# Bonus sums of the first two chunks: two columns of u per head pair in 32-column strips, in place of 96 spread columns

## The reference, cut to what matters

```python
for t in range(S):
    cur = np.einsum('bhd,bhe->bhde', u[None] * kt, vt)
    y[:, :, t] = np.einsum('bhd,bhde->bhe', rt, state + cur)
    state = wt[:, :, :, None] * state + np.einsum('bhd,bhe->bhde', kt, vt)
```

## Time and profile before

| | us |
|---|---|
| median of three runs | 647.96 |
| the profiled execution | 647.89 |
| its span in the trace | 646.1 |
| PE busy | 639.0 (99%) |
| DVE busy | 418.1 (65%) |
| ACT busy | 238.2 (37%) |
| POOL busy | 295.6 (46%) |

### The profile page before, as it was taken

The page is one execution under the profiler, slowest core; times in us unless marked ns, Lnnn a source line. Parts: engine busy times, 40 slices in busy tenths (PEclk is TensorE's granted clock), DMA queues, the critical chain, the costliest instruction groups (busy, mean ns, idle before and its releaser), DMA issues.

```text
span 646.1 us, 13797 instructions
## 1 busy us (share of the span) xinstructions
PE 639.0 (99%) x5044; PEld 592.0 (92%) x5044; DVE 418.1 (65%) x786; ACT 238.2 (37%) x561; POOL 295.6 (46%) x370
## 2 busy tenths in 40 slices
PE   8999999999999999999999999999999999999998
PEld 5998999877788888999999999999999999999997
DVE  7888988965357666655565656565656565656564
ACT  4776555645445554222222222222222222222221
POOL 5897424420499999996019900019900019000000
PEclk9999999999999999999999999999999999999999
DMA  8953454300000133100012100012100011001011
GB/s 323 403 196 131 137 167 175 121 18 1 1 2 1 56 102 99 40 1 1 1 50 98 50 1 0 1 49 98 50 1 0 0 50 50 0 1 49 0 50 50
DMA packets 19043, 42.34 MB, mean 66 GB/s; under 512 B 2608, under 2 KB 8752, under 8 KB 18992
## 3 DMA queue, kind: packets, MB, share of 16 engines
q1 hardware_dynamic: 18704, 41.23, 18.5%
q10 hardware_dynamic: 288, 0.39, 0.2%
HBM read 37.16 MB, written 4.46 MB: 64 GB/s over the span
## 4 chain that ended last, share of the span: by engine, by line
PE 89%; POOL 5%; DVE 3%; issue 1%; DMA 0%; ACT 0%; POOLq 0%; DVEq 0%
PE bank L1351 29%; PE bank L1352 28%; PE bank L1353 28%; POOL w_lo L549 4%; PE bank L1197 1%; PE bank L1266 1%; DVE fr L870 1%; PE bank L1278 1%; DMA rkw<-rkw_dram 0%; DVE att L928 0%; DVE fr L889 0%; PE bank L1222 0%; POOL tok L530 0%; DVE bank L1001 0%; PE bank L1286 0%
## 5 line engine op out<-in xcount | busy, mean ns | idle before, releaser
L1351 PE MATMUL bank<-x_lo,w_hi 128*128 128x256 f32 (+2 forms) x416 | 138.2, 332 | 0.6 <-DVE w_lo L971 0.3
L1352 PE MATMUL bank<-x_hi,w_lo 128*128 128x256 f32 (+2 forms) x416 | 135.2, 325 | 0.0
L1353 PE MATMUL bank<-x_hi,w_hi 128*128 128x256 f32 (+2 forms) x416 | 135.2, 325 | 0.0
L1352 PE MATMUL bank<-w_hi,g_lo 128*128 128x384 f32 x384 | 129.6, 337 | 0.0
L1353 PE MATMUL bank<-w_hi,g_hi 128*128 128x384 f32 x384 | 129.3, 337 | 0.0
L1351 PE MATMUL bank<-w_lo,g_hi 128*128 128x384 f32 x384 | 129.0, 336 | 0.0
L833 ACT ACTIVATE g_hi<-bank 128x512 fp32r<-128x512 f32 x96 | 57.5, 599 | 144.3 <-DVE bank L1057 122.4
L1351 PEld LDWEIGHTS bank<-x_lo,w_hi 128*128 128x128 f32 x416 | 78.2, 188 | 10.6 <-issue 2.6
L1353 PEld LDWEIGHTS bank<-x_hi,w_hi 128*128 128x128 f32 x416 | 78.3, 188 | 7.4
L1352 PEld LDWEIGHTS bank<-x_hi,w_lo 128*128 128x128 f32 x416 | 78.3, 188 | 7.1
L1050 DVE TENSOR_TENSOR u_sum<-p_copy,bank 128x256 f32<-128x256 f32 x56 | 23.6, 421 | 92.1 <-ACT p_copy L757 91.4
(11 more groups left out here) (133 smaller groups left out, 1259.6 us busy)
## 6 DMA issues: line engine op xcount, KB each, us to landing
raw<-w_dram SPq DMA_DIRECT2D x48, 384.0 KB, 3.7
rkw<-rkw_dram SPq DMA_DIRECT2D x10, 772.5 KB, 4.5
tok<-tok_dram SPq DMA_DIRECT2D x10, 576.0 KB, 6.2
k_blocks_dram<-k_blocks SPq DMA_DIRECT2D x8, 256.0 KB, 4.1
kt_sb<-k_blocks_dram SPq DMA_DIRECT2D x32, 64.0 KB, 2.0
out_dram<-acc SPq DMA_DIRECT2D x10, 192.0 KB, 1.9
rkw<-rkw_dram SPq DMA_DIRECT2D x2, 512.0 KB, 4.5
rkw<-rkw_dram SPq DMA_DIRECT2D x2, 260.5 KB, 3.2
```

The costliest lines, as they stand in the source:

```text
L1351: pe.matmul(out, wh, ml, start=start, stop=False, skip_group_check=shared)
L1352: pe.matmul(out, wl, mh, start=False, stop=False, skip_group_check=shared)
L1353: return pe.matmul(out, wh, mh, start=False, stop=stop, skip_group_check=shared)
```

## The change

`u_blk` and `u_col` go, and with them the four activations on ACT and the semaphore `s_ub`. In their place stands `u_heads`, two columns for each head pair: the first head's u with zeros below, the second's with zeros above. The same two DMAs now write into it. PE's `bonus` takes for each pair four products with 32 tokens' columns of `rk` as weights and the two columns of `u_heads`; each gives 32 partitions of the bank. The bank thus holds each head's sum once (8 columns), and `bonus_v` reads it 48 times over through a broadcast.

```diff
-            u_col = sb("u_col", [P, PAIRS], scope=scope)
-            u_blk = sb("u_blk", [P, PAIRS, PD], scope=scope)
+            u_heads = sb("u_heads", [P, PAIRS, 2], scope=scope)
...
-        s_ub = sem("s_ub")
...
-        blocks = const[:, C_BLK:C_BLK + PD]
...
             for o in range(2):
-                u_heads = bass.AP(u_d.tensor, o * D, [[1, D], [PD, PAIRS]])
-                sp.dma_start(u_col[64 * o:64 * o + D, :], u_heads, allow_slow_non_contiguous=True).then_inc(s_uc, 16)
+                u_half = bass.AP(u_d.tensor, o * D, [[1, D], [PD, PAIRS]])
+                sp.dma_start(u_heads[64 * o:64 * o + D, :, o], u_half, allow_slow_non_contiguous=True).then_inc(s_uc, 16)
...
-            pool.memset(u_col[:, :], 0.0).then_inc(s_zero, 1)
+            pool.memset(u_heads[:, :, :], 0.0).then_inc(s_zero, 1)
...
-            act.wait_ge(s_uc, 32)
-            act.wait_ge(s_const, 16)
-            for p in range(PAIRS):
-                act.activation(u_blk[:, p, :], blocks, ACT.Copy, scale=u_col[:, p:p + 1]).then_inc(s_ub, 1)
...
             def bonus_v(c, banks):
                 dve.wait_ge(s_pb, c + 1)
                 landed(dve, s_tok, c)
-                dve.tensor_tensor(bonus_v_sb[:, c % 2, :], v_of(c), banks["bonus"][:, 0:DM], ALU.mult).then_inc(s_cv, 1)
+                sums = banks["bonus"][:, 0:H].unsqueeze(2).broadcast_to([P, H, D])
+                dve.tensor_tensor(bonus_v_sb[:, c % 2, :].rearrange("p (h d) -> p h d", h=H),
+                                  v_of(c).rearrange("p (h d) -> p h d", h=H), sums, ALU.mult).then_inc(s_cv, 1)
...
             def bonus(c, banks):
 
                 pe.wait_ge(s_raw_rk[c], 1)
-                pe.wait_ge(s_ub, PAIRS)
+                pe.wait_ge(s_uc, 32)
                 if c == 1:
                     pe.wait_ge(s_kt, 1)
                 for p in range(PAIRS):
-                    ins = pe.matmul(banks["bonus"][:, p * PD:(p + 1) * PD], rk[:, c, p * CH:(p + 1) * CH], u_blk[:, p, :],
-                                    start=True, stop=True)
+                    for i in range(P // STRIP):
+                        rows, first = slice(STRIP * i, STRIP * i + STRIP), p * CH + STRIP * i
+                        ins = pe.matmul(banks["bonus"][rows, 2 * p:2 * p + 2], rk[:, c, first:first + STRIP],
+                                        u_heads[:, p, :], start=True, stop=True)
                 ins.then_inc(s_pb, 1)
```

## The result

The changed kernel takes 649.07 us, median of 14 runs (648.34 to 650.26), against 647.88 (647.74 to 648.05) for the kernel before in 14 runs beside them: a ratio of 1.0019 [1.0011, 1.0027]. The forecast was 647.6, with 648.6 as the upper end of its range. So the sign was wrong, and the time lies 0.5 us outside the range; in the band of 0.2% that the prediction calls "the same" it is just inside.

A forecast was written before the change was run, and what follows sets the result against it. The prediction took the chain POOL, then DVE, then PE from 67.19 us as the bound. Of 0.70 us saved on PE, 0.50 passes `scores` and 0.36 POOL's diagonal: 647.96 - 0.36 = 647.6 us, range 646.9 to 648.6.

The forecast's parts named there:

- the same: Whole kernel: a time within 0.2%, about 1.3 us, of the kernel before, given a chance of 0.89.
- The clock: TensorE's granted clock: at its upper level in all 40 slices, so no part of the change was priced at the slower one.
- ACT's activations, `const`, the clearing, at 0: Prologue: dropping ACT's 1.17 us of activations, loading `const` whole and clearing 8 columns on POOL each change nothing.
- Chunk 0's products, worth 0: PE, 10.21 to 11.34: shortening these products gains 0 to 0.05 us, taken as 0, because DVE sets the start of `values_even`.
- 32 records at 11.4 ns, 0.37 us: PE's chunk 1 bonus products: the new form takes 0.37 us in place of 1.07, moving `scores` 0.50 us earlier.
- `bonus_v` through a broadcast, 0: DVE's `bonus_v`: reading the sums through a broadcast costs 0; upper bound a doubling, 2 x 0.545 us more.
- From there each step follows the previous one: From `scores` of chunk 1 to the first layer: everything runs 0.50 us earlier, the first `up` at 16.99 in place of 17.49.
- far dearer products: Rival on PE's bonus products: a record costs 0.134 us as in the wide form, 654.3 us; chance 0.05 including another loss.
- POOL's wait vanishes and 0.36 us reaches the end: POOL's diagonal of chunk 2: starts at 36.70 in place of 37.06, and the kernel's end moves by the same 0.36 us.
- swallowed on the way: Rival: POOL's wait at 37.06 isn't cleared, or the strips run one after the other, 648.0 us; chance 0.22.
- a realigned POOL: Rival: DVE meets POOL's pieces at other moments, one more piece caught costing 0.98 us, 648.6 us; chance 0.14.
- dear products or another loss: The remaining case, a bonus record price as in the wide form or some other loss, outside the range; chance 0.05.

The follow-up runs named there:

- e2: The changed kernel with one product of 128*128 weights and two columns for each head pair, in place of four strips: 648.92 us, 1.0029 of the kernel before.
- e3: The changed kernel with strips of 64 columns, two products for each head pair in place of four: 649.86 us, 1.003 of the kernel before.
- e8: As e2, but each product reads the two columns of u through a broadcast, 96 moving columns: 647.85 us, 1.0001 of the kernel before.
- e1: The kernel before with 24 tiny strip products of zeros ahead of chunk 0's products, 96 PE instructions more: 648.47 us, 1.0012 of the kernel before.
- e7: The kernel before with 48 tiny products in place of e1's 24, 192 PE instructions more: 650.18 us, 1.0044 of the kernel before.
- e5: The changed kernel with SP holding weight slices 3 to 7 and all behind until chunk 1's bonus products are done: 650.60 us, 1.0044 of before.
- e10: The changed kernel; SP holds slices 4 to 7 until chunk 1's bonus is done, chunk 2's load precedes slice 7, ACT casts slice 4 after chunk 1's x: 649.12 us.
- e11: As e9, but chunk 1's bonus in strips of 32 columns, and scores of chunks 0 and 1 by 128 keys a product: 648.09 us, 1.0003 of before.
- e4: The changed kernel with SP holding weight slices 4 to 7 and all behind until POOL's first r * k is done: 649.19 us, 1.0023 of before.
- e9: As e8, but chunk 1's products in strips of 64 columns, each with 96 moving columns: 648.28 us, 1.0005 of the kernel before.
- e6: As e2, with a filling product of 512 columns behind chunk 0's products and one of 256 behind chunk 1's: 650.98 us, 1.0034 of before.

## Why the prediction was right or wrong, step by step

**The clock.** "No part of the change is priced at the slower level": right for the change as it stands. All runs of after are at 0.999 or more. In e2 and e3, with the same two columns in fewer products, half the runs are not.

**ACT's activations, `const`, the clearing, at 0.** Right: e8 has all these edits and measures 647.85 beside 647.87.

**Chunk 0's products, worth 0.** Right: `values_even` starts at 11.33 in after and 11.41 in before, a shift that the start of the products at 10.12 against 10.21 already has.

**32 records at 11.4 ns, 0.37 us.** Right: 0.34 us (11.76 to 12.10). The estimate from the Trainium skill, "TensorEngine Tiling", Performance Considerations, 0.80 us, is more than twice what the row shows, so on four strips the trace disagrees with its 60 cycles a product. `scores` was forecast at 13.12 with a shift of 0.50 and came at 13.04, released by DVE.

**`bonus_v` through a broadcast, 0.** Right. Both take 1.01 us, and in DVE's timeline of after:

```profile
12.90 1.01 DVE L944 TENSOR_TENSOR bonus_v_sb<-tok,bank 128x384 f32<-128x384 f32 x2
```

**"From there each step follows the previous one", first `up` at 16.99.** This step failed. It went from PE's operands alone and counted the time of the new products but not their number. 96 more PE instructions bring PE to the end of its loaded code at 16.4 rather than 19.7, before the next packet has come, and it stands still for 1.57 us in the profiled execution. e1 shows this without the change, e7 moves it, e5 and e10 remove it, and in e10 the first `up` is then at 16.98. The "far dearer products" rival looked for the loss in the price of a record; the records were cheap, and their number was dear.

**POOL's wait vanishes and 0.36 us reaches the end.** The first half held and the second failed, where it could be tested. In e11 the wait has gone and the diagonal is 0.31 us sooner. But of these only 0.04 is left at the next diagonal and 0.07 at 67, since POOL's work between the two diagonals got longer, by 0.23 and 0.32 us. The prediction took POOL's pieces as fixed in length. In after the wait grew instead, to 2.29 us, and the diagonal came at 38.87; the prediction had named a diagonal later than 37.06 as a sign that it was wrong. Its rival "swallowed on the way" has the outcome right, with 648.0 against e11's 648.09, and the reason it gives, that POOL and DVE slow each other when they meet, fits; that their meeting makes the longer pieces was not isolated and stays argued. So does whether the two longer low parts of DVE in after are a case of the rival "a realigned POOL", on the other engine.

**How the sum comes to +1.2.** In the profiled execution: 0.55 earlier at `update`, 1.57 of standstill, so some 1.0 later at the first `up` (0.98); 0.8 more by 38 us, while DVE's low parts take longer; and 0.6 at the DMA wait at 107.74 (1.83 at 101.18 us becomes 2.41 at 108.22). That is 2.4, and the spans differ by 2.3. The median of the runs is 1.2 above before, so a usual execution loses less than the profiled one. In e1, which has the instructions without the change, it is 0.6, of which the first `up` shows 0.53, PE's 67.34 only 0.15, and the rest comes with the DMA wait. So the standstill is shown as what breaks the forecast at the first `up`; how it becomes 1.2 us at the end is shown in part. How much of it is standstill, and how much the later stretch, only one trace tells, and that of the slowest run. What sets off the later growth and the new DMA wait is open.

**The range and the chances.** The range ended at 648.6, with a realigned POOL. Nothing in it stood for the loading of code, and the chance of 0.05 for "dear products or another loss" lay outside it. The chance of 0.89 for "within 0.2%" was right by the narrowest margin: the interval reaches to 0.27%.

## What to carry to other kernels

Count instructions as well as time where an engine executes new code in its first microseconds and the DMA engines are full: look in the DMA view for the instruction queue's packets, find which record the engine will reach when the next one comes, and read a wait on "issue" in the middle of one line as code that has not arrived. Splitting a product makes it quick but costs instructions. After narrowing one, look at the granted clock of the lines behind it in all the runs, not only in the profiled one. And a gain handed to an engine that is fixed in place is a gain only if its pieces keep their length: compare the durations of the same pieces, not just the waits.

## What the runs showed of the hardware

- **Code arrives by DMA, and no semaphore of the program tells of it.** The first packet of the instruction queue behind PE's start has 16 KiB, and PE stood still by 0.40 to 1.57 us until 1.4 to 1.6 us after its end, in five of the thirteen changed kernels (after, e1, e4, e7, e9), at a place that moves with the instruction count. Without queued data the packet began at 12.27 (e5) and 12.28 (e10), otherwise between 13.63 and 16.94, never before PE had started 125 product records; what sets the delay is open. The Trainium skill, "Runtime: NRT & Kernel Launch", Instruction fetch mechanics, says that the memory for instructions is refilled in blocks of 16 KiB by a DMA queue of the sequencer's own while the present block executes, and that the cost of it is mostly hidden. The packet's size agrees; "mostly hidden" doesn't, by the 1.57 us in after.
- **Strip products with two columns are issued at 11 ns a record.** 32 records of 128*32 weights and 2 columns took 0.34 us to the next line's start, with 96 columns 0.67 (e11, 11.81 to 12.48). With weights of 128*128 and the same 2 columns, 8 records take 1.05 us (e2), little less than with 96 (1.13, e8): fewer columns saved time in strips, and hardly any without.
- **Behind products of two columns the clock fell.** In two traces, after eight records of 128*128 weights and a filling product (e6), or sixteen of 128*64 (e3), `scores` ran at a granted clock of 0.50 and 0.53 and took 1.99 and 1.98 us in place of 1.10. The mean clock was at 0.997 or less in 5 of 10 executions of e2, 5 of 10 of e3 and 7 of 10 of e6, and in none of the ten of e8, with 96 columns. It isn't shown for every such kernel: all 14 of after, with two columns in strips, are at 0.999 or more.
